# Four unused arrays that move where the rounded tokens and their sums start in SBUF

## The reference, cut to what matters

```python
# 1. windowed attention: each query sees itself and the 63 keys before it
scores = (q @ k.T) / 8                      # per head, masked outside the window
attn = exp(scores - max) / (sum + 1e-9)
x = attn @ v                                # 1152 x 512
# 2. four experts, each token takes all four, weighted by p = probs / sum(probs)
for e in range(4):
    out += p[:, e] * (maximum(x @ w1[e], 0) @ w2[e])      # 512 -> 1024 -> 512
# 3. one layer with a cosine
h = out @ w_in                              # 512 -> 2048
result = (h * cos(h)) @ w_out               # 2048 -> 512
```

## Time and profile before

| what | value |
|---|---|
| median of 3 runs | 640.38 us (640.38 to 641.29) |
| the profiled execution | 639.62 us |
| its span, first to last instruction | 637.7 us |
| TensorE matmuls busy | 629.2 us, 99% of the span |
| VectorE, ScalarE, GpSimd busy | 48%, 41%, 43% |
| DMA, mean | 58 GB/s |

### The profile page before, as it was taken

One profiled execution on the slowest core, in us unless ns is written; L12 is line 12 of the kernel. 1 busy time (PEld: TensorE's weight loads), 2 busy tenths in 40 slices (PEclk: granted clock), 3 DMA queues, 4 the chain that ended last, 5 costly groups with the idle time before them and its releaser, 6 DMA issues.

```text
span 637.7 us, 10145 instructions
## 1 busy us (share of the span) xinstructions
PE 629.2 (99%) x3656; PEld 561.9 (88%) x3656; DVE 305.2 (48%) x722; ACT 260.3 (41%) x554; POOL 272.2 (43%) x404
## 2 busy tenths in 40 slices
PE   7999999999999999999999999999999999999998
PEld 5887899999989998989998888989999999999996
DVE  6754431215433315433315433426775666766564
ACT  6776322233321223321223321246655467544542
POOL 6783246698720296720296720287000059400000
PEclk9999999999999999999999999999999999999999
DMA  9874100022120011220012120033100012001011
GB/s 285 273 226 151 44 1 1 1 56 77 67 66 1 1 66 66 66 66 0 1 66 67 67 66 1 26 107 100 34 0 1 1 38 96 1 0 49 0 51 50
DMA packets 21896, 37.25 MB, mean 58 GB/s; under 512 B 2784, under 2 KB 14048, under 8 KB 21856
## 3 DMA queue, kind: packets, MB, share of 16 engines
q1 hardware_dynamic: 20688, 36.71, 17.7%
q10 hardware_dynamic: 1168, 0.02, 0.1%
HBM read 34.36 MB, written 2.36 MB: 58 GB/s over the span
## 4 chain that ended last, share of the span: by engine, by line
PE 96%; DVE 1%; POOL 1%; ACT 1%; issue 0%; DVEq 0%
PE bank L1166 31%; PE bank L1194 31%; PE bank L1225 16%; PE bank L1211 14%; PE bank L1158 2%; PE bank L1122 1%; PE bank L1142 1%; PE bank L1308 1%; DVE s_sb L823 1%; PE bank L1350 1%; POOL w_lo L424 0%; ACT prob L574 0%; DVE acc L973 0%; POOL prob L450 0%; DVE prob_t L838 0%
## 5 line engine op out<-in xcount | busy, mean ns | idle before, releaser
L424 POOL TENSOR_TENSOR w_lo<-w_raw,w_hi 128x128 fp32r<-128x128 f32 (+1 forms) x252 | 150.6, 633 | 214.4 <-ACT w_hi L606 211.9
L1166 PE MATMUL bank<-x_hi,w_hi 128*128 128x384 f32 (+1 forms) x384 | 131.2, 342 | 0.5 <-POOL w_lo L424 0.5
L1166 PE MATMUL bank<-x_hi,w_lo 128*128 128x384 f32 (+1 forms) x384 | 129.1, 336 | 0.0
L1166 PE MATMUL bank<-x_lo,w_hi 128*128 128x384 f32 (+1 forms) x384 | 128.7, 335 | 0.0
L1194 PE MATMUL bank<-w_hi,hp_hi 128*128 128x512 f32 x288 | 114.7, 398 | 0.1
L1194 PE MATMUL bank<-w_hi,hp_lo 128*128 128x512 f32 x288 | 113.4, 394 | 0.0
L1194 PE MATMUL bank<-w_lo,hp_hi 128*128 128x512 f32 x288 | 112.1, 389 | 0.0
L926 DVE TENSOR_TENSOR h_raw<-bank,h_raw 128x384 f32<-128x384 f32 x84 | 46.6, 555 | 91.9 <-PE bank L1211 91.9
L1166 PEld LDWEIGHTS bank<-x_hi,w_hi 128*128 128x128 f32 x384 | 72.1, 188 | 3.6 <-POOL w_lo L424 0.8
L1166 PEld LDWEIGHTS bank<-x_lo,w_hi 128*128 128x128 f32 x384 | 72.2, 188 | 1.5
L857 DVE SCALAR_TENSOR_TENSOR hp_lo<-bank,hp_hi 128x384 fp32r<-128x384 f32 x48 | 26.5, 556 | 98.1 <-ACT hp_hi L638 57.5
(11 more groups left out here) (103 smaller groups left out, 966.4 us busy)
## 6 DMA issues: line engine op xcount, KB each, us to landing
w_raw<-in_weights SPq DMA_DIRECT2D x43, 512.0 KB, 3.7
q_t<-in_q SPq DMA_DIRECT2D x12, 192.0 KB, 4.3
result<-acc SPq DMA_DIRECT2D x9, 256.0 KB, 2.0
w_raw<-in_weights SPq DMA_DIRECT2D x8, 256.0 KB, 5.8
k_t<-in_k SPq DMA_DIRECT2D x8, 224.0 KB, 5.3
v_w<-in_v SPq DMA_DIRECT2D x4, 384.0 KB, 5.0
v_w<-in_v SPq DMA_DIRECT2D x4, 320.0 KB, 6.5
k_t<-in_k SPq DMA_DIRECT2D x4, 192.0 KB, 3.7
```

What stands on the lines that cost most here:

```text
L424: last = nc.gpsimd.tensor_tensor(w_lo[:, f, at:at + part], raw[:, at - begin:at - begin + part], w_hi[:, f, at:at + part], ALU.subtract)
L1166: last = nc.tensor.matmul(ps[:, 0:TOK], w[:, f, chunk(c)], x[:, c, token_cols(t)], start=c == 0 and i == 0, stop=c == DC - 1 and i == 2)
```

## The change

Four arrays that nothing reads or writes are declared ahead of the tokens, the hidden values, `t` and `ex`. They hold 16, 48, 16 and 48 float32 numbers per partition: 64, 192, 64 and 192 bytes.

```diff
         w_raw = sb("w_raw", [P, STAGE, 2 * DM])
+        sb("before_x", [P, 16])
         x_hi = sb("x_hi", [P, DC, N], F32R)
         x_lo = sb("x_lo", [P, DC, N], F32R)
         p_tok = sb("p_tok", [P, E, TILES])
         half_pi = sb("half_pi", [P, 1])
+        sb("before_hp", [P, 48])
         hp_hi = sb("hp_hi", [P, HP, TOK], F32R)
         hp_lo = sb("hp_lo", [P, HP, TOK], F32R)
...
+            sum_sb("before_t", 16)
             t_hi = sum_sb("t_hi", 3, 2, TOK)
             t_lo = sum_sb("t_lo", 3, 2, TOK)
+            sum_sb("before_ex", 48)
             ex_hi = sum_sb("ex_hi", GROUPS, EX * P)
             ex_lo = sum_sb("ex_lo", GROUPS, EX * P)
```

## The result

The changed kernel takes 642.32 us (median of 8 runs, 641.49 to 642.77) against 640.4 us before. The ratio is 1.0028 with a 95% interval of 1.0018 to 1.0037. The forecast was 636.9 us, a gain, so the sign was wrong. The time lies inside the full range of 629.5 to 645.5 us, on the slow side that was kept for a loss in the up matmuls.

What follows compares the result with a forecast made beforehand. TensorE's own spacings, not waits or transfers, were taken to bound the kernel. Terms of -2.7 - 0.8 = -3.5 us, made on 639.62 and carried to the 640.38 median, gave 636.9 us; full range 629.5 to 645.5.

Steps and rivals of the forecast that it cites:

- What bounds the kernel: Whole kernel: the sum of TensorE's own spacings sets the end, busy 629.2 of 637.7 us; waits and transfers do not enter.
- Up and pair matmuls, -2.7 us: 1656 matmuls streaming tokens or token sums: at the down matmul's 1.073 of column time, 0.1717 us each, 2.7 us less.
- The fixed surplus (+3.8): Same 1656 matmuls, other reading: 15.6 ns over the columns in place of 13.3, 2.3 ns more each, 3.8 us more.
- The disturbed matmuls, -0.8 us: Where down products turn into up products: distance +64 on both sides removes about half the disturbance, 0.8 us gain (0 to 2).
- Down matmuls, "keep both residues, so nothing": Down matmuls of 512 columns: operand residues unchanged, so spacing stays at 0.2289 us and the time changes by nothing.
- Slower: First columns of every up and pair matmul: moving read hits the load once more, 2.3 ns each, 644.2 us; chance 0.32.
- Nothing changes: TensorE spacings: surplus comes from switching stationary operands or the rounded type, not addresses; 640.4 us; chance 0.24.
- The larger gain of 11 us: Up and pair matmuls: distance 0 may be the worst, half of the 13.3 ns surplus goes, 629.4 us; chance 0.15.
- The two rules: TensorE matmuls: issue-gap rule allows saving 17.9 us, an estimate of 622.5; independent-ports rule makes distance meaningless, 640.4 us.

## Why the prediction was wrong, point by point

**What bounds the kernel** was right. TensorE's spacings set the end, and no cover was lost: no new TensorE wait appeared.

**Up and pair matmuls, -2.7 us: failed.** The step carried the down product's ratio of 1.073 over to the up product, for having the same distance. The settled up spacing stayed at 0.1733 at distance 64. The fixed surplus (+3.8) failed as well, since the spacing didn't rise. A surplus read from one shape of matmul couldn't be carried to another: at equal distance 0 both have 13.3 ns (0.1733 and 0.2267), at distance 64 one has 13.3 and the other 15.6 or 20.

**The disturbed matmuls, -0.8 us: right in sign, too small, and for a reason that the runs refute.** The up matmuls gained 2.1 us, just over the upper end of 2. The first sixes behind down stretches hold 1.5 of it; the rest went from other places in the up runs. The prediction tied the disturbance to a change of distance at the turn. With all distances at 0 the first six still take 1.06. With tokens at 192 and hidden values at 192 or 0, where the distance between up and down products does change, they take 1.04 or 1.05. The prediction also misread a row. Its six pair products of 1.07 (268.90 to 269.97) are the last six before a down stretch and not the first behind one, so disturbances are not bound to the turn into up products.

**Down matmuls, "keep both residues, so nothing": this is the step that turned the sign.** They cost 3.7 us. Their own distance was the same, but more of their stretches took the upper of two paces, 0.2333 in place of 0.2289, and which one a stretch takes is settled at its start, behind the up run. That moving tokens and sums alone does it is shown; by what state is not. The rows for it stood in the prediction. The disturbed sixes were taken as proof that a run remembers what came before, and then the memory was allowed to act in one direction only, from down to up. The prediction held that a moved down spacing would make the distance the wrong measure. It is not wrong but incomplete: the common shift of 64 bytes left everything as it was.

**The rivals.** "Slower" named the right sign and the wrong place, the start of every up matmul. "Nothing changes", with two reads that never meet, is refuted as a reading of the surplus by the 640.54 to 636.27 us that 64 bytes on tokens and sums made. The larger gain of 11 us was seen nowhere. The best of 15 layouts tried, 636.27, is 4.1 us under the kernel before.

**The two rules.** A spacing of columns over 2.4 plus about 2.5 ns, which the Trainium skill gives as the gap of an isolated matmul (TensorE: Matmul & The Clock Gate, Back-to-back issue gap) and the prediction took for a stream with loads, was reached by no layout: the lowest settled surplus here is 13.3 ns. The Trainium skill's rule that TensorE's two read ports are independent (SBUF — State Buffer, Who interferes with whom) does not fit these runs as it stands. With nothing changed but start addresses the same matmul takes 0.2267, 0.2289, 0.2328 or 0.2333, with the next load running beside it.

**What stays open.** Why a distance of 64 bytes is neutral for the settled up matmuls, one of 32 or 128 is not and one of -64 only in places, what the state is physically, and whether the last 13.3 ns can be removed. That the load and the moving read disturb each other fits every run, since a common shift changes nothing, but no run took the load away.

## What to carry to other kernels

Where TensorE is the bound and its spacings exceed the columns by several per cent, start addresses are worth a scan, since two 64-byte moves (tokens with their sums, and hidden values) gave 0.65% here. Scan them together and not one after another: the same move of the tokens was +0.28% with one residue of the hidden values and about -0.7% with the other. Judge by the spacing over whole stretches of both kinds of matmul, since a change to one kind can be paid for by the kind behind it.

## What the runs showed of the hardware that was not expected

- One pair of arrays at fixed addresses has two steady paces, 0.687 and 0.700 us per three matmuls. Stretches of eighteen hold either, and which one is settled at their start: by the up run before them, and in one place of both kernels by a late start.
- Up runs at a distance of -64 have three paces in one trace, 0.1763, 0.1750 and 0.1733 us.
- A distance of 32 bytes is the costliest seen for up matmuls: 0.1767 us per 384 columns, against 0.1733 at 0 and 64 and 0.1758 at 128.
- Shifts by 256 and 512 bytes changed nothing (639.93 us against 640.4), and one common shift of all arrays by 64 changed nothing (642.30 against 642.32).
